# The cubic of a rational activation by completing the square, with |h| made on two engines by turns

## The reference

```
h = x @ w_in                                   # 24960 x 128 times 128 x 2048
P = a[0] + a[1] * h + a[2] * h*h + a[3] * h*h*h
Q = 1.0 + abs(b[0]) * abs(h) + abs(b[1]) * h*h
g = P / (Q + 1e-06)
return g @ w_out                               # 24960 x 2048 times 2048 x 128
```

## Time and profile before

| what | value |
|---|---|
| median of 3 runs | 2366.12 us (2360.96 to 2369.22) |
| the profiled execution: span, first to last instruction | 2364.7 us |
| the profiled execution: time around its span | not given by itself; the median of the runs is 1.4 us above the span |
| third stage, first to last `activation` start | 738.9 us to 2357.1 us |
| busy in the span: TensorE, VectorE, ScalarE, GpSimd | 88%, 86%, 84%, 80% |

### The profile page before, as it was taken

The page is one execution under the profiler, slowest core; times in us unless marked ns, Lnnn a source line. Parts: engine busy times, 40 slices in busy tenths (PEclk is TensorE's granted clock), DMA queues, the critical chain, the costliest instruction groups (busy, mean ns, idle before and its releaser), DMA issues.

```text
span 2364.7 us, 33272 instructions
## 1 busy us (share of the span) xinstructions
PE 2081.2 (88%) x8964; PEld 1464.9 (62%) x8964; DVE 2042.7 (86%) x2499; ACT 1993.8 (84%) x2670; POOL 1892.7 (80%) x1218
## 2 busy tenths in 40 slices
PE   7888578889877999999999999999999999999997
PEld 5666478889874555555555555555555555555554
DVE  3777566767666999999999999999999999999998
ACT  3677455555546999999999999999999999999998
POOL 3666367777755888888888888888888888888887
PEclk9999889999997999999999999999999999999999
DMA  6888655656552111111111111111111111111100
GB/s 163 246 257 263 206 128 146 154 139 162 137 127 60 29 29 28 28 31 28 31 48 28 28 28 28 28 28 28 31 28 32 48 28 28 28 28 28 28 11 11
DMA packets 65724, 175.02 MB, mean 74 GB/s; under 512 B 5046, under 2 KB 8414, under 8 KB 62686
## 3 DMA queue, kind: packets, MB, share of 16 engines
q1 hardware_dynamic: 65694, 174.67, 28.0%
HBM read 102.89 MB, written 71.76 MB: 74 GB/s over the span
## 4 chain that ended last, share of the span: by engine, by line
DVE 22%; ACT 20%; issue 11%; POOL 9%; PE 7%; ACTq 0%; DVEq 0%; DMA 0%; POOLq 0%
DVE g_s L735 9%; DVE lin L723 8%; ACT lin L634 6%; POOL den L609 6%; ACT mag L640 5%; ACT r_p L652 5%; DVE num L727 4%; PE m_p L790 3%; PE h_p L811 3%; POOL slope L601 3%; ACT den L645 3%; DVE xy_lo L714 1%; ACT xy_hi L625 0%; DVE oT L743 0%; ACT o_s L681 0%
## 5 line engine op out<-in xcount | busy, mean ns | idle before, releaser
L609 POOL TENSOR_TENSOR den<-slope,mag 128x832 f32<-128x832 f32 x480 | 944.6, 1968 | 43.4 <-POOL slope L601 6.9
L822 PE MATMUL acc_p<-g_s,w_out_s 128*128 128x416 f32 x1920 | 759.6, 518 | 18.3 <-DVE g_s L735 15.0
L601 POOL TENSOR_SCALAR slope<-mag,den_c 128x832 f32<-128x832 f32 x480 | 500.0, 1042 | 168.0 <-ACT mag L640 154.5
L723 DVE SCALAR_TENSOR_TENSOR lin<-lin,coef,h_p 128x832 f32<-128x832 f32 x480 | 516.4, 1076 | 33.9 <-ACT mag L640 33.9
L727 DVE SCALAR_TENSOR_TENSOR num<-lin,coef,h_p 128x832 f32<-128x832 f32 x480 | 518.8, 1081 | 17.0
L811 PE MATMUL h_p<-xy_hi,w_lo 128*128 128x416 f32 x960 | 406.5, 423 | 132.4 <-DVE num L727 110.2
L735 DVE SCALAR_TENSOR_TENSOR g_s<-num,coef,r_p 128x832 f32<-128x832 f32 x480 | 515.3, 1074 | 3.5 <-issue 1.8
L822 PEld LDWEIGHTS acc_p<-g_s,w_out_s 128*128 128x128 f32 x1920 | 346.9, 189 | 233.5 <-issue 210.8
L634 ACT ACTIVATE lin<-h_p,coef 128x832 f32<-128x832 f32 x480 | 458.0, 954 | 5.2 <-PE h_p L811 5.2
L645 ACT ACTIVATE den<-den 128x832 f32<-128x832 f32 x480 | 434.8, 906 | 27.4 <-POOL den L609 26.1
L811 PEld LDWEIGHTS h_p<-xy_hi,w_lo 128*128 128x128 f32 x960 | 180.7, 188 | 399.8 <-DVE num L727 384.2
(11 more groups left out here) (66 smaller groups left out, 2878.1 us busy)
## 6 DMA issues: line engine op xcount, KB each, us to landing
bent<-bent_s SPq DMA_DIRECT2D x60, 576.0 KB, 4.7
bin_s<-bent SPq DMA_DIRECT2D x24, 1440.0 KB, 12.6
x_s<-in_x SPq DMA_DIRECT2D x60, 416.0 KB
back<-back_s SPq DMA_DIRECT2D x24, 960.0 KB, 6.5
vin_s<-back SPq DMA_DIRECT2D x30, 768.0 KB, 5.8
v_s<-in_v SPq DMA_DIRECT2D x30, 416.0 KB
out<-o_s SPq DMA_DIRECT2D x60, 208.0 KB
pos_s<-in_pos_emb SPq DMA_DIRECT2D x30, 88.0 KB
```

Source lines behind the costliest of these rows:

```text
L601: nc.gpsimd.tensor_scalar(slope[:, q % DEEP], mag[:, q % DEEP], den_c[:, 1:2], den_c[:, 0:1], ALU.mult, ALU.add).then_inc(slope_done, 1)
L609: nc.gpsimd.tensor_tensor(den[:, q % DEEP], slope[:, q % DEEP], mag[:, q % DEEP], ALU.mult).then_inc(den_done, 1)
L723: nc.vector.scalar_tensor_tensor(out=lin[:, q % 2], in0=lin[:, q % 2], scalar=coef[:, 2:3], in1=h, op0=ALU.add, op1=ALU.mult).then_inc(qua ...
L822: mm = nc.tensor.matmul(acc_p[:, 0:TOK], w_out_s[:, ft], g_s[:, q % DEEP, t], start=(ft == 0), stop=(ft == FT - 1))
```

## The change

The cubic is divided by its leading coefficient, and completed to a square: (((h + c)^2 + l) * h + p0) with c = a2/(2 a3) and l = a1/a3 - c^2, and a3 is multiplied into the output weights instead. So ScalarE makes (h + c)^2 straight from PSUM (Square with a per-partition bias), and VectorE makes num = (square + l) * h in one pass where there were two. `activation` uses p0 = a0/a3. |h| of even pairs stays an Abs on ScalarE, ahead of the square; |h| of odd pairs is made on VectorE, by clearing the sign bit, ahead of the numerator and behind a wait for the square. The coefficients are worked out once, by 12 small VectorE instructions at the start of the stage, and ScalarE scales w_out (128 x 2048) once. The square has 2 buffers.

```diff
+            LEAD_H, LEAD_E, DEEP, NUMS, SQUARES = 5, 3, 4, 8, 2
...
                 def slopes(i, q):
                     G = i * PER + q
-                    pool.wait_ge(mag_done, G + 1)
+                    if q % 2:
+                        pool.wait_ge(mag_dve, i * (PER // 2) + q // 2 + 1)
+                    else:
+                        pool.wait_ge(mag_act, i * (PER // 2) + q // 2 + 1)
...
-                def line(i, q):
-                    G = i * PER + q
-                    act.wait_ge(h_done, G + 1)
-                    if positive(G - 1):
-                        act.wait_ge(num_done, G - 1)
-                    nc.scalar.activation(lin[:, q % 2], h_p[:, q % 2, :, 0:TOK], ACT.Copy, scale=coef[:, 3:4]).then_inc(lin_done, 1)
+                def magnitude(i, q):
+                    G = i * PER + q
+                    act.wait_ge(h_done, G + 1)
                     if positive(G - DEEP + 1):
                         act.wait_ge(den_done, G - DEEP + 1)
-                    nc.scalar.activation(mag[:, q % DEEP], h_p[:, q % 2, :, 0:TOK], ACT.Abs).then_inc(mag_done, 1)
-
+                    nc.scalar.activation(mag[:, q % DEEP], h_p[:, q % 2, :, 0:TOK], ACT.Abs).then_inc(mag_act, 1)
+
+                def squared(i, q):
+                    G = i * PER + q
+                    act.wait_ge(h_done, G + 1)
+                    if positive(G - SQUARES + 1):
+                        act.wait_ge(num_done, G - SQUARES + 1)
+                    nc.scalar.activation(square[:, q % SQUARES], h_p[:, q % 2, :, 0:TOK], ACT.Square, bias=centre[:]
+                                         ).then_inc(square_done, 1)
+
+                def from_h(i, q):
+                    if q % 2 == 0:
+                        magnitude(i, q)
+                    squared(i, q)
...
                 nc.scalar.activation(den_c[:], den_raw[:], ACT.Abs).then_inc(coef_ready, 1)
+                act.wait_ge(cubic_ready, 1)
+                nc.scalar.activation(w_out_k[:], w_out_s[:], ACT.Copy, scale=lead[:, 3:4]).then_inc(w_scaled, 1)
...
                     reciprocal(i, q)
                     if ahead:
-                        line(i + (q + LEAD_E) // PER, (q + LEAD_E) % PER)
-                        magnitude(i + (q + LEAD_E) // PER, (q + LEAD_E) % PER)
+                        from_h(i + (q + LEAD_E) // PER, (q + LEAD_E) % PER)
...
-                def numerator(i, q, between=lambda: None):
-
+                def numerator(i, q):
                     G = i * PER + q
                     h = h_p[:, q % 2, :, 0:TOK]
-                    dve.wait_ge(mag_done, G + 1)
-                    nc.vector.scalar_tensor_tensor(out=lin[:, q % 2], in0=lin[:, q % 2], scalar=coef[:, 2:3], in1=h,
-                                                   op0=ALU.add, op1=ALU.mult).then_inc(quad_done, 1)
-                    between()
-                    dve.wait_ge(quad_done, G + 1)
-                    nc.vector.scalar_tensor_tensor(out=num[:, q % NUMS], in0=lin[:, q % 2], scalar=coef[:, 1:2], in1=h,
+                    dve.wait_ge(square_done, G + 1)
+                    if q % 2:
+                        if positive(G - DEEP + 1):
+                            dve.wait_ge(den_done, G - DEEP + 1)
+                        nc.vector.tensor_scalar(mag[:, q % DEEP].bitcast(I32), h.bitcast(I32), NO_SIGN, None,
+                                                ALU.bitwise_and).then_inc(mag_dve, 1)
+                    nc.vector.scalar_tensor_tensor(out=num[:, q % NUMS], in0=square[:, q % SQUARES], scalar=level[:], in1=h,
                                                    op0=ALU.add, op1=ALU.mult).then_inc(num_done, 1)
...
-                    nc.vector.scalar_tensor_tensor(out=g_s[:, q % DEEP], in0=num[:, q % NUMS], scalar=coef[:, 0:1],
+                    nc.vector.scalar_tensor_tensor(out=g_s[:, q % DEEP], in0=num[:, q % NUMS], scalar=ratio[:, 0:1],
                                                    in1=r_p[:, :, 0:TOK], op0=ALU.add, op1=ALU.mult).then_inc(act_done, 1)
...
-                        mm = nc.tensor.matmul(acc_p[:, 0:TOK], w_out_s[:, ft], g_s[:, q % DEEP, t], start=(ft == 0),
+                        mm = nc.tensor.matmul(acc_p[:, 0:TOK], w_out_k[:, ft], g_s[:, q % DEEP, t], start=(ft == 0),
                                               stop=(ft == FT - 1))
...
                 for q in range(LEAD_H):
                     hidden(0, q)
+                pe.wait_ge(w_scaled, 1)
```

More of the change, by code:

```diff
@@ L22 @@
 F32R = mybir.dt.float32r
+I32 = mybir.dt.int32
 ALU = mybir.AluOpType
@@ L45 @@
 EPS = 1e-6
+LEAST, TINY = 1e-6, 1e-30
+NO_SIGN = 0x7FFFFFFF
 assert ROWS * J == SEQ and J_BLOCKS % SLOTS == 0 and K_BLOCKS % SLOTS == 0
@@ L528, in hyena_mlp @@
             ITERS = J_BLOCKS // SLOTS
-            LEAD_H, LEAD_E, DEEP, NUMS = 5, 3, 4, 8
+            LEAD_H, LEAD_E, DEEP, NUMS, SQUARES = 5, 3, 4, 8, 2
             HALF = JB // 2
@@ L538, in hyena_mlp @@
             den_c = sb("den_c", [128, 2])
-            lin = sb("lin", [128, 2, 2, TOK])
+            size = sb("size", [128, 4])
+            lead = sb("lead", [128, 4])
+            ratio, half_sq = sb("ratio", [128, 3]), sb("half_sq", [128, 2])
+            centre, level = sb("centre", [128, 1]), sb("level", [128, 1])
+            w_out_k = sb("w_out_k", [128, FT, D])
+            square = sb("square", [128, SQUARES, 2, TOK])
             mag = sb("mag", [128, DEEP, 2, TOK])
@@ L552, in hyena_mlp @@
             coef_ready, pool_passed = sem("coef_ready"), sem("pool_passed")
+            coef_step, cubic_ready, w_scaled = sem("coef_step"), sem("cubic_ready"), sem("w_scaled")
             vin_in, x_in = sems("vin_in"), sems("x_in")
@@ L555, in hyena_mlp @@
             hi_done, lo_done = sem("hi_done"), sem("lo_done")
-            h_done, lin_done, mag_done = sem("h_done"), sem("lin_done"), sem("mag_done")
-            quad_done, num_done, slope_done, den_done = sem("quad_done"), sem("num_done"), sem("slope_done"), sem("den_done")
+            h_done, square_done = sem("h_done"), sem("square_done")
+            mag_act, mag_dve = sem("mag_act"), sem("mag_dve")
+            num_done, slope_done, den_done = sem("num_done"), sem("slope_done"), sem("den_done")
             log_done, r_done, act_done, used = sem("log_done"), sem("r_done"), sem("act_done"), sems("used", DEEP)
@@ L627, in split_hi @@
                                          ACT.Copy).then_inc(hi_done, 1)
-                def line(i, q):
+                def magnitude(i, q):
                     G = i * PER + q
                     act.wait_ge(h_done, G + 1)
-                    if positive(G - 1):
-                        act.wait_ge(num_done, G - 1)
-                    nc.scalar.activation(lin[:, q % 2], h_p[:, q % 2, :, 0:TOK], ACT.Copy, scale=coef[:, 3:4]).then_inc(lin_done, 1)
-                def magnitude(i, q):
-                    G = i * PER + q
                     if positive(G - DEEP + 1):
                         act.wait_ge(den_done, G - DEEP + 1)
-                    nc.scalar.activation(mag[:, q % DEEP], h_p[:, q % 2, :, 0:TOK], ACT.Abs).then_inc(mag_done, 1)
+                    nc.scalar.activation(mag[:, q % DEEP], h_p[:, q % 2, :, 0:TOK], ACT.Abs).then_inc(mag_act, 1)
[10 more added lines that the diff above has]
+                    squared(i, q)
                 def logarithm(i, q):
@@ L658, in _ @@
                 for q in range(LEAD_E):
-                    line(0, q)
-                    magnitude(0, q)
+                    from_h(0, q)
                 logarithm(0, 0)
@@ new lines, in cubic @@
+                def cubic():
+                    nc.vector.tensor_scalar(size[:].bitcast(I32), coef[:].bitcast(I32), NO_SIGN, None, ALU.bitwise_and).then_inc(coef_step, 1)
+                    dve.wait_ge(coef_step, 1)
+                    nc.vector.tensor_tensor(half_sq[:], size[:, 0:2], size[:, 2:4], ALU.max).then_inc(coef_step, 1)
+                    dve.wait_ge(coef_step, 2)
+                    nc.vector.tensor_tensor(lead[:, 0:1], half_sq[:, 0:1], half_sq[:, 1:2], ALU.max).then_inc(coef_step, 1)
+                    dve.wait_ge(coef_step, 3)
+                    nc.vector.tensor_scalar(lead[:, 1:2], lead[:, 0:1], LEAST, TINY, ALU.mult, ALU.add).then_inc(coef_step, 1)
+                    nc.vector.tensor_scalar(size[:, 0:1], coef[:, 3:4], 0.0, 2.0, ALU.is_ge, ALU.mult).then_inc(coef_step, 1)
+                    dve.wait_ge(coef_step, 5)
+                    nc.vector.tensor_tensor(lead[:, 2:3], size[:, 3:4], lead[:, 1:2], ALU.max).then_inc(coef_step, 1)
+                    dve.wait_ge(coef_step, 6)
+                    nc.vector.scalar_tensor_tensor(out=lead[:, 3:4], in0=size[:, 0:1], scalar=-1.0, in1=lead[:, 2:3],
+                                                   op0=ALU.add, op1=ALU.mult).then_inc(coef_step, 1)
+                    dve.wait_ge(coef_step, 7)
+                    nc.vector.reciprocal(size[:, 1:2], lead[:, 3:4]).then_inc(coef_step, 1)
+                    dve.wait_ge(coef_step, 8)
```

(9 more changed lines are left out.)

## The result

The changed kernel took 2455.07 us (median of 4 runs, 2454.84 to 2461.05), the kernel before 2366.55 us in 4. The ratio is 1.0392, with a 95% interval of 1.0371 to 1.0413: slower by 3.9% (the two medians alone divide to 1.0374, inside the interval). The prediction was 2448 us, range 2345 to 2500.

What follows compares the result with a forecast made beforehand. ScalarE, VectorE and a ScalarE-GpSimd loop were taken to bound the kernel together. The change's odd-pair loop, 3.55 us a pair against 3.378, over 479 steps adds 82 us to 2366.1: 2448 us, range 2345 to 2500.

Steps and rivals of the forecast that it cites:

- The loop over odd pairs: Slope, den, logarithm, reciprocal, activation, VectorE's mag, back to GpSimd's slope: 7.10 us for two pairs, 3.55 a pair.
- activation to mag: Loop term on VectorE, from the activation's start to the next VectorE instruction: 0.99 us.
- the hand-over to GpSimd: Loop term from the end of VectorE's mag until GpSimd's slope starts: 0.21 us, between 0.08 and 0.3.
- reciprocal to activation: Loop term from ScalarE's reciprocal to the VectorE activation that waits for it: 0.93 us.
- The extra instructions hide: Small extra ScalarE and VectorE instructions fit into time the loop leaves idle; at worst 30 us in all.
- Setup covered: Stage start: 12 small VectorE instructions, 7 us, and w_out's scaling, 1.9 us, hidden behind loads; uncovered up to 9 us.
- Square: ScalarE's Square takes line's place and line's time, 0.95 us, as both have a per-partition operand.
- Rival A, throughput decides: GpSimd never waits for an odd mag and sets the pace, 3.17 us a pair: 2266 us; chance 0.15.
- Rival B, a fast mag: VectorE makes |h| at two elements a step, about 0.6 us; 3.33 a pair, 2345 us; chance 0.07.
- Rival C, no change: Loop terms some 0.35 us smaller in sum, 3.38 us a pair: 2366 us; chance 0.05.
- Rival D: Much slower: Square needs table loads in each pair, or TensorE loses its clock of 1.00; above 2850 us; chance 0.02.
- The reading of the kernel before: ScalarE, VectorE and a loop through ScalarE and GpSimd, 3.31 us a pair, lie within 0.07 of the pace, 3.378.

Runs made afterwards that it cites:

- e3: Changed kernel with VectorE's odd mag moved behind the instruction that makes num, TensorE's next h waiting for both: 2687.01 us, ratio 1.138 to the kernel before.
- e5: As e4, but VectorE runs the numerator of q+3 before the mag of q+4: 2262.9 us, ratio 0.9577 to the kernel before.
- e6: Changed kernel with |h| of every pair on VectorE, behind activation and square, none on ScalarE: 2458.11 us, ratio 1.0406 to the kernel before.
- e4: Changed kernel with VectorE's odd mag made for pair q+4 behind the activation, waiting for h; ScalarE's odd square waits for that mag: 2303.11 us.
- e2: Changed kernel with VectorE's odd mag moved ahead of the activation, its waits for square and den kept: 2535.99 us, ratio 1.0747 to the kernel before.
- e1: Changed kernel with |h| of every pair on ScalarE ahead of the square, none on VectorE: 2311.29 us, ratio 0.9796 to the kernel before.

## Why the prediction was right, and where it was off

The mechanism came as forecast: a loop over the odd pairs, through VectorE's list, and not the busiest engine. That the total came so close is in part luck, as the second point shows.

- *The loop over odd pairs*, 7.10 us: 7.09 in the turn shown. In that turn its terms stand as written: mag 1.018 us where 1.04 was taken, activation to mag 1.00 (0.99), the hand-over to GpSimd 1716.10 - (1714.87 + 1.02) = 0.21 (0.21), reciprocal to activation 0.94 (0.93). e3, e5 and e6 show it as a cause: +0.97 us for a step put into it, the gain once the mag is out of it (e4 and e5), and in e6 no price for more passes that don't make it longer.
- *The extra instructions hide*: nearly, and one link was too small. Measured is 2 x 3.574 = 7.148 us on average, 0.05 more than the 7.10 of the sum. From 1200 to 2200 us the trace has 139 turns, and in them every link but one agrees with its term within 0.02 us. The one is reciprocal to activation, for which 0.93 was taken from the stage's first pair: it averages 1.00. It takes 0.94 in every second turn, in which the activation's pair is q = 2, 6, 10 or 14 of its block (0.93 to 0.95 in all 69), and 1.03 to 1.16 in the 70 others, in which q is divisible by four. At two of the four places of either kind xy or xy_lo stands just ahead of the activation. Here are the activations of the second kind, behind the oT copy and behind xy, and then one of the first kind behind xy_lo:

```profile
1705.58 0.59 DVE L787 COPY oT<-acc_p 128x416 f32<-128x416 f32 x1 [0.28 <-PE acc_p L868]
1706.78 1.08 DVE L779 SCALAR_TENSOR_TENSOR g_s<-num,ratio,r_p 128x832 f32<-128x832 f32 x1 [0.60 <-ACT r_p L671]
...
1720.26 0.69 DVE L726 TENSOR_TENSOR xy<-m_p,x_s 104x512 f32<-104x512 f32 x1 [0.67 <-PE m_p L836]
1721.07 1.08 DVE L779 SCALAR_TENSOR_TENSOR g_s<-num,ratio,r_p 128x832 f32<-128x832 f32 x1
...
1726.62 0.58 DVE L733 TENSOR_TENSOR xy_lo<-m_p,xy_hi 128x416 fp32r<-128x416 f32 x1
1728.17 1.08 DVE L779 SCALAR_TENSOR_TENSOR g_s<-num,ratio,r_p 128x832 f32<-128x832 f32 x1 [0.96 <-issue]
```

  Their reciprocals start at 1705.74, 1720.03 and 1727.23, so the distances are 1.04, 1.04 and 0.94. An extra instruction ahead is thus not enough to make the link longer. What makes it so isn't shown; the pairs divisible by four also share one buffer of g_s. The mag, 0.02 too large in the sum, gave a little back. All in all the pace was 0.024 a pair above 3.55, 11 us; the earlier start of the stage gave half of it back, which is luck, and the forecast came out 7 us low.
- *Setup covered*: right. The small instructions took 0.14 to 0.23 us each (0.58 was the upper bound taken), and the copy of w_out 2.00 us, from 703.84 to 705.84, ahead of ScalarE's first xy_hi at 713.33.
- *Square*: 0.941 us where 0.95 was taken. The rule of the Trainium skill ("ScalarE: Activation LUTs", What ACT_TABLE_LOAD costs), about 93 ns for a pointer operand, fits: 941 - 847 (the Abs of this kernel) = 94 ns.
- *Rival A, throughput decides*: wrong for this order. e5 came out at 3.176 a pair, 2263 us, which is almost the 3.17 and 2266 that the rival was given, but that is partly luck. The 3.17 was mis-sized: GpSimd behind itself takes 3.08 (1709.01 to 1712.09), since in the earlier trace rows 0.08 us lay between the end of its den and the next slope. So e5 isn't quite at GpSimd's limit. Its waits, num for the square and the square for the mag, fit the loop square, num, mag as the rest; no run tests that. The same error made the idle time ahead of odd slopes come out at 0.98 us where about 0.7 was predicted.
- *Rival B, a fast mag*: out. It took 1018 ns for 832 elements from PSUM, as 32-bit integers, where 1040 was read off rows at the plain rate. Of the Trainium skill's page "VectorE: DVE Perf Modes", the section "Why PSUM operands drop a tier", which says 1x for fp32, is thus the one that fits this operation; the tier table's "at most 2x" is a cap, and this operation gets nothing of it.
- *Rival C, no change*: out. Its smaller terms, a mag of 0.8 and a hand-over of 0.08, measured 1.02 and 0.21.
- *Rival D*: out. Two table loads in the whole run, as before, and a granted clock of 1.00. But the mechanism on TensorE's side exists: e2 and e3, with longer gaps, ran at 0.93 to 0.97.
- *The reading of the kernel before*, with ScalarE, VectorE and the loop within 0.07 us of the pace of 3.378: too close. Only the loop's 3.31 is; ScalarE's is 3.29 by its own sum and 3.274 in e1, about 0.1 below.

## What to carry to other kernels

When several engines work in order on one stream, ask of every moved instruction not how busy its new engine is, but what stands ahead of it in that engine's list, and whether that in turn waits for something the moved instruction feeds. Sum such a loop from start-to-start distances of the timeline and divide by the number of items it advances; compare that with the busiest engine. Here the same work gave 2455, 2303 or 2263 us by the place of one pass and its waits, and in the slowest of the three the engine it was moved to had 22% of the stage free.

## What the runs showed of the hardware that was not expected

TensorE's granted clock fell inside a steady stage in the two runs with the longest gaps: its longest wait for g_s was 2.3 us in e2 and 2.2 in e3, and at most 1.6 in the others. The runs with a pace of 3.73 and 4.06 us had 0.93 to 0.97 over the stage's stretches, those of 3.57 and less 1.00. It isn't the last gap alone that decides: in e2 a project behind 2.30 us of idle time took 3.14 us, in e3 one behind 2.21 us took 1.66, and of the 44 in e2 from 1200 to 2200 us that stood behind more than 2 us, 15 took over 2 us and 29 did not.

```profile
1707.65 1.66 PE L870 MATMUL acc_p<-g_s,w_out_k 128*128 128x416 f32 x4 [2.21 <-DVE g_s L779]
```

So a longer loop can slow an engine that has time to spare. In e2 that reached ScalarE, and in e3 it cost nothing.

ScalarE's durations don't give its pace when its queue is full. In e1 an Abs reads 1.42 us and a square 1.52 on average, against 0.85 and 0.94 in the changed kernel, yet the starts lie 0.74 and 0.84 us apart, close to the 0.75 and 0.84 of the earlier trace rows:

```profile
1700.36 1.41 ACT L644 ACTIVATE mag<-h_p 128x832 f32<-128x832 f32 x1
1701.10 1.51 ACT L651 ACTIVATE square<-h_p,centre 128x832 f32<-128x832 f32 x1
1701.94 1.45 ACT L660 ACTIVATE den<-den 128x832 f32<-128x832 f32 x1
```
